# Where one half-tile's split stands in VectorE's program: ahead of or behind the ordering of the expert runs, in the first step of the second expert layer

## What is computed

```python
logits = x @ w_gate; noise_scale = np.log1p(np.exp(x @ w_noise))
noisy_logits = logits + noise_scale * noise
top2 = np.argpartition(-noisy_logits, 2, axis=1)[:, :2]
...
for e in range(E):
    for k in range(2):
        mask = top2[:, k] == e
        h = np.maximum(x[mask] @ w1[e], 0.0)
        out[mask] += top2_w[mask, k, None] * (h @ w2[e])
```

## Time and profile before

| | |
|---|---|
| time, median of 3 runs | 985.99 us (985.29 to 988.22) |
| time of the profiled execution | 981.03 us |
| its span | 979.2 us |
| mean granted TensorE clock | 0.968 of full |
| busy: TensorE | 918.4 us (94%) |
| busy: VectorE | 554.1 us (57%) |
| busy: GpSimd | 423.3 us (43%) |
| busy: ScalarE | 258.5 us (26%) |

### The profile page before, as it was taken

The page is one execution under the profiler, slowest core; times in us unless marked ns, Lnnn a source line. Parts: engine busy times, 40 slices in busy tenths (PEclk is TensorE's granted clock), DMA queues, the critical chain, the costliest instruction groups (busy, mean ns, idle before and its releaser), DMA issues.

```text
span 979.2 us, 22988 instructions
## 1 busy us (share of the span) xinstructions
PE 918.4 (94%) x7093; PEld 882.1 (90%) x7094; DVE 554.1 (57%) x1247; ACT 258.5 (26%) x493; POOL 423.3 (43%) x460
## 2 busy tenths in 40 slices
PE   5999999899889989999689999999999999999995
PEld 4888888899889989988689999999999999999995
DVE  8888989667754545648583544425335344443532
ACT  2222333124322323424220222203122231321210
POOL 7333333424655554446553343433434434344232
PEclk9999998989989999989899999999999999999998
DMA  8787899305411111123424534425333444513223
GB/s 266 229 263 256 268 353 359 111 3 188 169 34 51 33 34 41 42 98 93 139 66 90 131 96 115 111 44 117 104 52 101 121 104 112 112 32 54 45 48 51
DMA packets 61848, 115.96 MB, mean 118 GB/s; under 512 B 14352, under 2 KB 42192, under 8 KB 61776
## 3 DMA queue, kind: packets, MB, share of 16 engines
q1 hardware_dynamic: 39552, 75.37, 23.1%
q0 software_dynamic: 18336, 34.91, 17.2%
q10 hardware_dynamic: 3888, 4.80, 1.4%
HBM read 83.63 MB, written 31.51 MB: 118 GB/s over the span
## 4 chain that ended last, share of the span: by engine, by line
PE 78%; DVE 10%; issue 5%; POOL 2%; DMA 2%; DVEq 1%; ACT 1%; another core or an unknown queue 0%; ACTq 0%; SPq 0%; POOLq 0%
PE ps L1894 21%; PE ps L1895 20%; PE ps L1896 20%; PE ps L1841 3%; PE ps L1796 2%; PE ps L1800 2%; PE ps L1765 2%; PE ps L1742 2%; PE ps L1827 2%; PE ps L1854 1%; PE ps L1790 1%; DVE grow L1042 1%; PE ps L1750 1%; DVE hid_lo L1557 1%; DVEq L388 1%
## 5 line engine op out<-in xcount | busy, mean ns | idle before, releaser
L1894 PE MATMUL ps<-x_hi,weights 128*128 128x256 f32 x984 | 282.2, 287 | 18.9 <-issue 12.3
L1895 PE MATMUL ps<-x_lo,weights 128*128 128x256 f32 x984 | 281.2, 286 | 2.1 <-issue 2.0
L1896 PE MATMUL ps<-x_hi,weights 128*128 128x256 f32 x984 | 280.6, 285 | 2.5 <-issue 2.4
L1894 PE MATMUL ps<-weights,hid_hi 128*128 (+1 forms) x616 | 220.0, 357 | 3.4 <-DVE hid_lo L1557 2.3
L1895 PE MATMUL ps<-weights,hid_hi 128*128 (+1 forms) x616 | 212.5, 345 | 0.8 <-issue 0.8
L1896 PE MATMUL ps<-weights,hid_lo 128*128 (+1 forms) x616 | 211.5, 343 | 0.0
L1894 PEld LDWEIGHTS ps<-x_hi,weights 128*128 128x128 f32 x984 | 189.0, 192 | 21.0 <-issue 20.5
L929 ACT ACTIVATE hid_hi<-ps 128x512 fp32r<-128x512 f32 x164 | 97.1, 596 | 411.9 <-PE ps L1896 373.5
L1557 DVE SCALAR_TENSOR_TENSOR hid_lo<-ps,hid_hi 128x512 fp32r<-128x512 f32 x164 | 112.1, 690 | 153.2 <-ACT hid_hi L929 130.1
L1895 PEld LDWEIGHTS ps<-x_lo,weights 128*128 128x128 f32 x984 | 189.1, 192 | 6.3 <-issue 6.2
L1896 PEld LDWEIGHTS ps<-x_hi,weights 128*128 128x128 f32 x984 | 189.0, 192 | 2.9 <-issue 2.9
(11 more groups left out here) (313 smaller groups left out, 1148.8 us busy)
## 6 DMA issues: line engine op xcount, KB each, us to landing
stage<-in_w_dram SPq DMA_DIRECT2D x18, 1536.0 KB
kv_in<-in_kv_T_dram SPq DMA_DIRECT2D x24, 512.0 KB, 5.8
kv_in<-in_kv_T_dram SPq DMA_DIRECT2D x24, 448.0 KB, 4.0
w_in<-in_w_T_dram SPq DMA_DIRECT2D x24, 258.5 KB, 4.6
moe_rows<-zeros SPq DMA_DIRECT2D x26, 192.0 KB, 4.0
out_dram<-zeros SPq DMA_DIRECT2D x26, 192.0 KB
x_rows<-y_tok ACTq DMA_DIRECT2D x24, 192.0 KB
w2T_raw<-in_w_T_dram SPq DMA_DIRECT2D x2, 1536.0 KB
```

Of the source, the lines that this page charges most:

```text
L1894: pe.matmul(out_ps, hi, by_hi, start=first, stop=False)
L1895: pe.matmul(out_ps, hi, by_lo, start=False, stop=False)
L1896: return pe.matmul(out_ps, lo, by_hi, start=False, stop=final)
```

## The change

In step 0 of the second layer, the split of the second tile of step 1 is written ahead of `second_order`, and no longer behind it. No instruction is added or taken away on any engine.

```diff
                         hidden_low(0, 2)
                         hidden_low(0, 3)
                         split_x(1, 1, 0)
+                        split_x(1, 1, 1)
                         second_order()
-                        split_x(1, 1, 1)
                         second_starts()
                         second_tables()
                         low_w2(dve.value_load(run_no[0:1, 1:2], min_val=2, max_val=E + 1))
```

## The result

The changed kernel took 988.33 us (median of 20 runs) and the kernel before 985.93 (20 runs). The two medians lie 2.4 us apart. So I take the cost as 0.4%. A range in parentheses behind a ratio is its 95% interval. The profiled execution took 984.49 us with a span of 982.7, against 981.03 and 979.2. The forecast was +2.7 us or +0.27%. The direction and the mechanism were right and the size was too small.

The account below looks back on a forecast made before the run. TensorE was taken to bound the kernel, with 78% of the chain. A later start of 1.2 us and 1.5 us of slow clock, nothing gained, gave +2.7 us: 988.7 against 985.99, with a range from 983.8 to 990.8.

Parts of the forecast that it names:

- The stall and its cause: End of step 0: TensorE idles 3.13 us for the split; GpSimd's L711 holds VectorE's L1381, an excess of 3.90 us.
- The stall moves: TensorE enters step 1 without a stop; its wait moves ahead of the down product, about 6 us long.
- The later start: Step 1's first down product starts 1.2 us later (0.4 to 1.4), because VectorE's chain ends later.
- that bound: If the hold catches second_order's first instruction, VectorE's chain there ends at 503.63, against 503.42 in the forecast case.
- the sentence that the chain was 0.3 us short of being the limit: Kernel before, step 1: second hidden_low ends at 512.36, the down product needing it starts at 512.66, about 0.3 us later.
- The slow clock: Behind the new wait the clock falls on step 1's down products, costing 1.5 us (0 to 3.0).
- the fourth rival: The slow clock lasts twice as long: 1.2 + 3.0 = 4.2 us, giving 990.2; chance 0.13.
- the stall's length is simply won: Rival: the stall is gone, TensorE gains 3.1 us and the slow stretch's 1.5, giving 981.4; chance 0.05.
- the hold costs nothing: Rival: GpSimd's subtraction no longer delays VectorE's chain; the down product starts 2.5 us early, 983.5 to 985.0; chance 0.10.
- there is no stall in most executions: Rival: in timed runs L1381 gets through, so the change costs 3.5 to 5.0 us, 989.5 to 991.0; chance 0.10.
- Other queues: GpSimd's gather starts 1.36 us later, low_w2 and SyncE's load move too; no cost, and nothing later gives the delay back.
- one of the prediction's own signs of being wrong: In the new trace, a gap of TensorE that ends with a table or a gather would count against the prediction.

Follow-up runs that it names:

- old order, L711 later: Kernel before, with GpSimd's subtraction L711 made behind the scatter of step 0 in the second layer; ratio 0.9971.
- new order, L711 later: Changed kernel, with GpSimd's subtraction L711 made behind the scatter of step 0 in the second layer; ratio 0.9999 over the kernel before.
- split in the middle: Kernel before, with the second tile's split put inside second_order, behind its eight short instructions and ahead of the two comparisons; L711 unmoved; ratio 1.0042.
- changed, TensorE kept busy: Changed kernel, with TensorE given 25 products on constants while it waits in step 1; ratio 1.0035 over the kernel before.
- new order, shorter chain: Changed kernel, with VectorE's low_w2 and loop_ends made in step 1, behind the split of step 2's second tile; ratio 0.9990 over the kernel before.
- old order, shorter chain: Kernel before, with VectorE's low_w2 and loop_ends made a step later, in step 1; ratio 0.9995.
- old order, both: Kernel before, with L711 moved behind the scatter of step 0 and low_w2 and loop_ends made in step 1; ratio 0.9953.
- before, once more: The kernel before, unchanged, run again for one more trace; D1 13.84 us and D2 18.13 us.
- old order, fill ahead of L711: Kernel before, with GpSimd filling an unused tile (1024 bf16 numbers a partition) just ahead of its subtraction L711; ratio 1.0012.
- changed, once more: The changed kernel, unaltered, run again on another chip; ratio 1.0052 over the kernel before.

## Why the forecast was right, and where it was too small

| kernel | D1 us | D2 us | D2 - D1 | ratio |
|---|---|---|---|---|
| before | 13.85 | 18.16 | 4.31 | 1 |
| changed | 15.53 | 22.21 | 6.68 | 1.0039 |
| old order, L711 later | 9.78 | 14.09 | 4.31 | 0.9971 |
| new order, L711 later | 11.69 | 17.55 | 5.86 | 0.9999 |
| split in the middle | 13.83 | 20.00 | 6.17 | 1.0042 |
| changed, TensorE kept busy | 15.50 | 19.78 | 4.28 | 1.0035 |
| new order, shorter chain | 12.15 | 18.96 | 6.81 | 0.9990 |
| old order, shorter chain | 12.31 | 16.57 | 4.26 | 0.9995 |
| old order, both | 8.96 | 13.22 | 4.26 | 0.9953 |
| before, once more | 13.84 | 18.13 | 4.29 | one run |
| old order, fill ahead of L711 | 12.71 | 18.58 | 5.87 | 1.0012 |
| changed, once more | 15.40 | 22.36 | 6.96 | 1.0052 |

The median of 988.33 us lies beside the forecast 988.7, but that nearness is luck. The forecast was +2.7 us, the traces show +4.05 and the ratio +3.8. The direction came as forecast, and so did the moved wait and the slow clock on the down products; both terms of the sum were too small. The prediction put its border between same and slower at 0.3%. The 0.39% measured lies above it, on the side to which it gave 0.42 and not 0.49, though the interval reaches to both sides.

**The stall and its cause.** Right. GpSimd's subtraction holds an instruction of VectorE and the chain behind it, and taking it away took 4.07 us out of D1. Not every instruction is held, which the prediction didn't say (see the last section).

**The stall moves.** Right. TensorE starts step 1 without a stop and waits in it until VectorE has gone through its chain.

**The later start.** Forecast 1.2 us (0.4 to 1.4), measured 1.68. Of the ways in which the hold could fall I took the one in which `second_order`'s first instruction gets away. It was the one caught, so the chain ended where I had put that bound (503.63; measured 503.66). Against the 503.42 of the sum that is 0.24 us, half of the miss. The other half is the step from `hidden_low` to the product: I took 0.14 us from another row, and it was 0.38 here (513.24 to 513.62). It was already 0.30 in the kernel before (512.36 to 512.66), which I had read as slack of VectorE's chain. It was none: 0.29 or 0.30 us pass there also in kernels whose trace shows TensorE waiting for `hidden_low`. So the sentence that the chain was 0.3 us short of being the limit was wrong, and the whole delay of the chain went into D1.

**The slow clock.** This is the term that was most off: forecast 1.5 us (0 to 3.0), measured 2.4 (6.68 - 4.31). The slow clock covered 5.0 us of down products, not 3.2. By this it lies nearer the fourth rival, which had 3.0 for this term and 4.2 in all; D2 grew by 4.05. The six traces in which TensorE waited in step 1 and wasn't kept busy, for 2.48 to 6.13 us in all, gave 1.6 to 2.7 us (D2 - D1 less 4.3). So it varies, and I had sized it by the one stretch that happened to stand beside the change.

**The other rivals.** That the stall's length is simply won is refuted by the two kernels in which it was removed and nothing gained. That the hold costs nothing, and that there is no stall in most executions, are not borne out: VectorE was held in every trace in which L711 stood at its place, eight of them. Three of these have the old order. How the runs without a trace went isn't shown.

**Other queues.** Right for the time, but one of the prediction's own signs of being wrong did show. GpSimd's gather (506.43) and everything behind it were later by the chain's delay, but step 1's first down product didn't wait for them. The 2.69 us ahead of the transposes, where the program waits for the tables and the gather, are a gap of that kind. The profile names no releaser for it. The tables were done at 507.83, and the transposes started 3.23 us after the first gather's instruction (3.25 with the shorter chain), so it was most likely the gather. This wait lies within the longer one for `hidden_low` and adds nothing to it. With the shorter chain it is what remains.

## What to carry to other kernels

A stall names the last thing that was late. Before moving that thing forward, look at what it is moved past: if the mover must wait at the new place, everything queued behind it waits too, and here that chain was already the limit itself, tied with TensorE. A short time between the end of one instruction and the start of the next isn't slack; compare it with a place where the one is known to wait for the other. Ask as well which work a slow clock after a wait will fall on. Here it cost nothing ahead of another wait, and its full length on the critical products. The better remedy lay one engine further, with the instruction that held VectorE: moved to a later place, where nothing critical meets it, it gave 0.3%, and 0.5% with the chain shortened.

## What the hardware showed that I had not expected

The hold begins before GpSimd's recorded start. In the changed kernel L1408 started at 495.31 and would have been over by 495.47, which is 0.41 us ahead of L711's 495.88, and it was caught. With the fill in front, a comparison that ended at 472.74, 0.95 us ahead of L711's 473.69, got through. So for instructions like these, with both inputs in SBUF, the point lies between 0.41 and 0.95 us ahead of the start in the record. GpSimd's last indirect DMA of the lists runs there too, but it alone doesn't hold them: in the kernel with the fill the same comparison ran beside it (GpSimd's L627, 471.81 to 472.77) in its usual 0.47 us. At the earlier pair of the earlier trace rows an instruction on one number, L1313, was over 0.01 us ahead of L711 and wasn't held, so the half microsecond isn't shown for every kind of instruction or every start of L711. How much of it is the record and how much the engine wasn't tried. By issue order and these records the rule of the Trainium skill ("SBUF — State Buffer", Who interferes with whom), that the one that issues first has the ports, would have let L1381 through in the kernel before and L1408 in the changed one. The measurement decides.

An instruction on 8 numbers is held like one on 304. L1408 with two inputs took 4.12 us and L1423 with one took 2.88, and both ended 0.04 or 0.05 us after L711.

Other instructions are not held at all. In the kernel with the fill the split's subtraction L1553, which reads PSUM and SBUF, ran from 473.87 to 474.43 in its usual 0.56 us, inside L711 (473.69 to 477.19). At the earlier pair of the earlier trace rows a sum with one input in PSUM got through inside L711, just ahead of the copy from SBUF to SBUF that was held:

```profile
442.84 0.17 DVE L1316 TENSOR_TENSOR row_pos<-ps,filled 128x16 f32<-128x16 f32 x1
```

All the instructions that were seen held have their inputs in SBUF. So work that reads PSUM, such as the split, can stand beside L711, as far as these rows go.
